# Three edits to the attention part of a mixer kernel: key products by head, queries turned by another engine, an earlier first attention product

## The chip, the cores and the metric

One core of a Trainium2 chip runs the kernel. The time is the device time of one execution, in microseconds (us); the median of three runs is given. Five engines work side by side and wait for each other by semaphores: TensorE (PE; its weight loads are shown apart as PEld), VectorE (DVE), ScalarE (ACT), GpSimd (POOL) and SyncE (SP), which issues the DMAs. Matrix products end in PSUM, which has eight banks of 2 KB in each of 128 partitions.

## The reference

Linear attention without a softmax feeds a mixer with a rotation (first mixer), which feeds a second mixer. There are 8 batches, 8 heads of 64 channels, and 576 tokens; all data are fp32.

```
kv  = einsum('bhsd,bhse->bhde', k, v)            # one 64x64 matrix per batch and head
out = einsum('bhsd,bhde->bhse', q, kv)
x   = out / sqrt(mean(out*out, -1) + 1e-6) * g_norm      # then (B, S, 512)

theta = x @ w_theta
y = w_tok_r @ (x*cos(theta)) + w_tok_i @ (x*sin(theta))  # over tokens
u = x + y
x2 = u + relu(u @ w_ch)

h = relu(x2.T @ w_tok1) @ w_tok2 ; u2 = x2 + h.T         # second mixer
out = u2 + relu(u2 @ w_ch1) @ w_ch2
```

## The kernel before

The program has four parts, one after the other: phase_a (attention and first mixer, batch by batch), and phase_b to phase_d (the second mixer). Only phase_a is touched, and one wait at the entry of phase_b. Each engine has its own hand-written list of instructions; what one engine issues it executes in that order, so a wait holds everything behind it on that engine.

Most products are made exact enough by splitting both operands into a high part (fp32r, made by ACT with a copy) and a low part (the difference, made by DVE or POOL) and adding three products: high by high, high by low, low by high (`split_matmul`, L40 to L44). The attention's own products and the transposes are plain fp32; in the trace a plain fp32 product is two pairs of a weight load and a pass, a transpose one pair.

Tokens come in five slices (four of 128, one of 64). In phase_a an engine's `body(b)` does batch b's mixer and, woven into it, batch b+1's attention. Body 0 (`first=True`) also prepares weights; bodies 1 to 6 are a loop, body 7 stands alone. On TensorE a body is, in order:

1. `theta(b, j)` for five slices (L281 on): x times w_theta, into banks that DVE empties (`fraction`, L653 on). From slice 2 on it waits until DVE has done the slice before last.
2. `kv(b+1)` (L229): for five slices and four pairs of heads one fp32 product of 128 by 128, into the bank `ps_kv`; of each only the two diagonal 64 by 64 blocks are used. DVE's `kv_copy` (L618) copies these into a block-diagonal tile (two copies), whose other blocks are zero. `kv_copy` stands on DVE after all of the batch's `fraction`, `magnitude` and `rotate`.
3. `q_transpose(b+1, 0)` (L245): four transposes of 128 by 128 of the queries, against the identity; ACT copies the bank out (`q_copy`, L469).
4. `token_mix_first_half(b)` (L352): the token products of four column groups, in five pairs of tiles (four of two, one of one). For each pair TensorE first waits for the high parts (`a_zhi`, ACT), does 16 products (8 in the last pair), then waits for the low parts (`g_zlo`, POOL's `z_lo`, L850) and does 8 (4).
5. `attend(b+1, 0)` (L257): four fp32 products of the turned queries (stationary) with the block-diagonal tile (moving), then `q_transpose(b+1, 1)`.
6. For the groups 4 to 7: `token_mix(b, g)` (27 products), `attend(b+1, g-3)`, and, but for the last, `q_transpose(b+1, g-2)`. `attend(n, j)` waits from j=2 on until DVE has done `norm(n, j-2)` (L634), because two banks take turns.
7. `channel_mix(b, g)` for eight groups (12 products each), with transposes of the new x between them (`x_transpose`, L268) and after them.

DVE meanwhile does, in its own order: `fraction`, `magnitude`, `rotate` of the five slices; `kv_copy`; for the groups 0 to 7 `residual` (two additions, L689 on), `u_lo`, and from group 3 on `mean_square` and from group 4 on `norm` of the next batch; then for the groups 0 to 7 `relu_add` (L706), with the transposes of the result (`turn_x2`, L714, 32 by 32 blocks inside 128 by 576), `norm` of slice 4 and `x_lo`. `mean_square(n, j)` waits for ACT's `squares(n, j)`, which stands behind `u_hi` on ACT. POOL raises the mean square to the power -1/2 and multiplies by g_norm (`inverse_rms`, `gain`).

SP issues in body b: `load_kv(b+2)`, which waits for kv(b+1), `load_q(b+2)` (five DMAs, rows of 256 B), which waits for the last `q_transpose` of batch b+1, the store of x2 and 16 DMAs that store the turned result in blocks of 32 by 32 (`store_turned`, rows of 128 B).

## Time and profile before

| | |
|---|---|
| time, median of 3 runs (range) | 1215.15 us (1215.12 to 1215.16) |
| the profiled execution's own time | 1213.61 us |
| its span, first to last instruction | 1211.8 us |
| granted TensorE clock, mean | 0.995 of 2.4 GHz |
| token products of phase_a on TensorE | until 553.9 us of the span |

The span leaves out 1.8 us that lie around the first and the last instruction. A row of the timeline gives the start, the length, the engine, the line of the code, the operation, what it writes and reads, the shape and the number of like instructions in a row; in brackets stands how long the engine sat idle before it and who released it. A product's length includes its way through the array, so products overlap in the rows: the pace of a series is (length of the row minus length of one) divided by (count minus 1).

### The profile page before, as it was taken

The page shows a single profiled execution, that of the slowest core. Times are in us where ns is not written, and L with a number is a line of the kernel's source. Part 1 is how long each engine was busy: PE and PEld are TensorE (multiplying, and loading weights), DVE is VectorE, ACT ScalarE, POOL GpSimd, SP SyncE. Part 2 cuts the span into 40 slices and gives each one's busy share as a digit, 9 for nine tenths or more (in the row PEclk, how much of TensorE's full clock was granted, in tenths as well). Part 3 has the DMA queues.
Part 4 walks back from the last instruction along what each step waited for, and adds up shares of the span by engine and source line. Part 5 has one row for each costly group of instructions (what it writes and reads, how often), then busy time and mean ns, then how long its engine had stood idle before and what let it go on. Part 6 is the DMA issues. An engine that isn't in the chain of part 4 may idle for free.

```text
span 1211.8 us, 20530 instructions
## 1 busy us (share of the span) xinstructions
PE 1182.7 (98%) x7590; PEld 1150.9 (95%) x7590; DVE 836.4 (69%) x1227; ACT 490.0 (40%) x764; POOL 338.2 (28%) x209
## 2 busy tenths in 40 slices
PE   6999999999999999999999899999999999999998
PEld 5899999999999999999898899999999899999998
DVE  3877778686868778678556566766766786666664
ACT  3532424242433324244433455555556543333331
POOL 4443534444252525440553042133210000000000
PEclk9999999999999999999999999999999999999999
DMA  9825445272543440036998587856669999989973
GB/s 254 172 53 112 79 94 101 39 156 39 111 76 86 78 107 10 34 87 227 344 300 295 164 332 267 298 201 263 248 233 334 382 304 300 271 240 308 290 189 53
DMA packets 348428, 228.12 MB, mean 188 GB/s; under 512 B 268880, under 2 KB 316368, under 8 KB 347344
## 3 DMA queue, kind: packets, MB, share of 16 engines
q1 hardware_dynamic: 348368, 227.32, 64.7%
q8 instruction: 38, 0.62, 0.2%
q14 instruction: 22, 0.18, 0.0%
HBM read 136.84 MB, written 92.80 MB: 189 GB/s over the span
## 4 chain that ended last, share of the span: by engine, by line
PE 91%; DMA 3%; DVE 2%; issue 1%; ACT 1%; SPq 1%; POOL 0%; DVEq 0%; POOLq 0%; ACTq 0%
PE bank L42 11%; PE bank L44 11%; PE bank L43 11%; PE bank L1267 10%; PE bank L1269 10%; PE bank L1268 10%; PE bank L309 6%; PE bank L314 6%; PE bank L308 6%; PE bank L240 3%; PE bank L265 3%; PE bank L279 1%; PE bank L253 1%; DMA attention_g<-g_scratch 1%; DMA qkv_x_tokens<-x_tokens_scratch 1%
## 5 line engine op out<-in xcount | busy, mean ns | idle before, releaser
L308 PE MATMUL bank<-weights_tok,z_z 128*128 128x288 f32 x576 | 164.2, 299 | 0.0
L309 PE MATMUL bank<-weights_tok,z_z 128*128 128x288 f32 x576 | 161.3, 295 | 0.0
L314 PE MATMUL bank<-weights_tok,z_z 128*128 128x288 f32 x576 | 124.8, 294 | 0.0
L309 PEld LDWEIGHTS bank<-weights_tok,z_z 128*128 128x128 f32 x576 | 108.2, 188 | 0.0
L308 PEld LDWEIGHTS bank<-weights_tok,z_z 128*128 128x128 f32 x576 | 108.1, 188 | 0.0
L838 POOL TENSOR_TENSOR weights_rms_inverse<-weights_mean_squares,weights_minus_half 128x8 f32<-128x8 f32 x40 | 65.5, 1639 | 129.6 <-DVE weights_mean_squares L632 129.3
L314 PEld LDWEIGHTS bank<-weights_tok,z_z 128*128 128x128 f32 x576 | 92.6, 188 | 0.0
L519 ACT ACTIVATE weights_x_channel_major<-attention_u 128x288 fp32r<-128x288 f32 x64 | 28.4, 444 | 139.4 <-DVE attention_u L699 138.8
L853 POOL TENSOR_TENSOR z_z<-tokens_cos,z_z 128x512 fp32r<-128x512 f32 x24 | 34.5, 1437 | 173.5 <-ACT z_z L512 173.5
L42 PE MATMUL bank<-weights_x_channel_major,weights_ch 128*128 128x288 f32 x256 | 77.2, 301 | 0.0
L43 PE MATMUL bank<-weights_x_channel_major,weights_ch 128*128 128x288 f32 x256 | 75.4, 294 | 0.0
L44 PE MATMUL bank<-weights_x_channel_major,weights_ch 128*128 128x288 f32 x256 | 75.4, 294 | 0.0
L1496 ACT ACTIVATE attention_staged<-bank 128x384 f32<-128x384 f32 x108 | 52.3, 489 | 36.1 <-PE bank L1269 31.3
L697 DVE TENSOR_TENSOR attention_u<-bank,weights_x_channel_major 128x288 f32<-128x288 f32 x64 | 29.1, 454 | 52.5 <-PE bank L314 52.4
L1267 PE MATMUL bank<-z_u_slot,weights_up 128*128 128x384 f32 x192 | 64.1, 334 | 0.0
L1268 PE MATMUL bank<-z_u_slot,weights_up 128*128 128x384 f32 x192 | 64.1, 334 | 0.0
L1269 PE MATMUL bank<-z_u_slot,weights_up 128*128 128x384 f32 x192 | 64.1, 334 | 0.0
L846 POOL TENSOR_TENSOR tokens_x_token_major<-attention_x_normed,weights_g_norm 128x512 f32<-128x512 f32 x40 | 52.7, 1326 | 0.0
L484 ACT ACTIVATE weights_x_channel_major<-bank 128x512 fp32r<-128x512 f32 (+1 forms) x40 | 21.6, 557 | 76.7 <-PE bank L279 76.7
L42 PE MATMUL bank<-weights_theta,weights_x_channel_major 128*128 128x512 f32 x128 | 51.0, 398 | 0.4 <-DVE weights_theta L735 0.4
L1549 DVE TENSOR_TENSOR attention_staged<-attention_staged 128x384 f32<-128x384 f32 x36 | 28.1, 781 | 32.7 <-ACT attention_staged L1496 32.5
L44 PE MATMUL bank<-weights_theta,weights_x_channel_major 128*128 128x512 f32 x128 | 50.0, 390 | 0.0
(287 smaller groups left out, 3697.7 us busy)
## 6 DMA issues: line engine op xcount, KB each, us to landing
g_scratch<-attention_staged SPq DMA_DIRECT2D x36, 960.0 KB, 5.0
weights_g<-g_scratch SPq DMA_DIRECT2D x24, 1152.0 KB, 10.3
g_scratch<-attention_staged SPq DMA_DIRECT2D x36, 384.0 KB, 5.6
x_scratch<-attention_u SPq DMA_DIRECT2D x8, 1152.0 KB, 4.5
u_scratch<-attention_u SPq DMA_DIRECT2D x8, 1152.0 KB, 6.2
weights_raw_u<-u_scratch SPq DMA_DIRECT2D x6, 1536.0 KB, 7.4
qkv_u_left<-u_scratch SPq DMA_DIRECT2D x12, 768.0 KB, 9.4
qkv_k<-in_k_dram SPq DMA_DIRECT2D x32, 256.0 KB, 4.9
```

The costliest lines, as they stand in the source:

```text
L42: eng.matmul(out, w[0], x[0], start=first, stop=False)
L43: eng.matmul(out, w[0], x[1], start=False, stop=False)
L44: return eng.matmul(out, w[1], x[0], start=False, stop=last)
L308: pe.matmul(out, x, wtok[0][:, zt, hs], start=(i == 0), stop=False)
L309: pe.matmul(out, x, wtok[1][:, zt, hs], start=False, stop=False)
L314: mm = pe.matmul(tok_bank(b, g)[:, 0:HALF], z[1][:, zt, c * P:(c + 1) * P], wtok[0][:, zt, half * HALF:(half + 1) * HALF], start=False, st ...
L838: gp.tensor_tensor(rms_inv[:, i, :], msq[:, i, :], minus_half[:, :], ALU.pow).then_inc(g_pow, 1)
L846: gp.tensor_tensor(xtm[:, j, :].rearrange("p (h e) -> p h e", h=H), xn[:, i, :].rearrange("p (h e) -> p h e", h=H), gn[:, :].unsqueeze(1). ...
L1267: eng.matmul(out, w[0], x[0], start=False, stop=False, skip_group_check=True)
L1268: eng.matmul(out, w[0], x[1], start=False, stop=False, skip_group_check=True)
L1269: return eng.matmul(out, w[1], x[0], start=False, stop=last, skip_group_check=True)
L1496: act.activation(tile(n, k), src, ACT.Relu).then_inc(done, 1)
```

## The change

- **Keys by head on column halves.** `kv` takes each head by itself: a weight load of 64 columns (k) and a product with 64 moving columns (v), even heads into partitions 0 to 63, odd heads into 64 to 127, of half as many columns of the bank. 40 fp32 products of half width take the place of 20. `kv_copy` makes four copies of 64 by 128 into two tiles, and stands on DVE behind slice 3's `magnitude` and slice 2's `rotate`, before slice 4's `fraction`.
- **Queries from batch 2 on turned by DVE.** `load_blocks` loads queries in 16 DMAs so that blocks of 32 by 32 lie in place, and `turn_q` turns them on DVE with four transposes of 128 by 576; in bodies 1 to 5 behind `relu_add` of the groups 1 to 4, in body 0 (for batch 2) at the very end of DVE's list. TensorE's `q_transpose` and ACT's `q_copy` stay for batches 0 and 1 alone. The turned queries have a tile for all five slices; `attend` reads 64 columns of it for the last slice.
- **First attention product between token pairs.** `attend(b+1, 0)` stands behind the second of the five pairs of `token_mix_first_half`, in the other of the two banks.
- In body 0 ACT's `q_copy(1, 0)` and the conversion of w_ch stand earlier. `squares` writes into a slice of `fraction`, one `x_normed` tile shares memory with `x_left`, so `sines` of slice 3 waits for the batch's last `theta`.

```diff
@@ sync
-        def load_q(n):
-            wait(sp, p_qt, NT * n)
-            for j in range(NT):
-                load_tile(qin, q, n, j, s_q)
+        def load_blocks(n):
+            if isinstance(n, int) and n == PE_TURNED:
+                sp.wait_ge(p_qt, NT * n)
+            else:
+                sp.wait_ge(d_q, HP * (n - PE_TURNED))
+            for hp in range(HP):
+                for part in range(PARTS):
+                    h, first = 2 * hp + part // 2, part % 2 * SIDE
+                    sp.dma_start(q_raw[part * SIDE:(part + 1) * SIDE, hp, :].rearrange("p (b d) -> p b d", d=SIDE),
+                                 q[n, h, :, first:first + SIDE].rearrange("(b s) d -> s b d", s=SIDE)
+                                 ).then_inc(s_q, DMA)
...
@@ tensor, kv
-                    hs = slice(2 * hp, 2 * hp + 2)
-                    mm = pe.matmul(ps_kv[:, hp * P:(hp + 1) * P], kin[:, j, hs, :].rearrange("p h d -> p (h d)"),
-                                   vin[:, j, hs, :].rearrange("p h d -> p (h d)"), start=(j == 0 and hp == 0),
-                                   stop=(j == NT - 1 and hp == HP - 1))
+                    for side in range(2):
+                        h = 2 * hp + side
+                        mm = pe.matmul(ps_kv[side * D:(side + 1) * D, hp * D:(hp + 1) * D], kin[:, j, h, :],
+                                       vin[:, j, h, :], start=(j == 0 and hp == 0),
+                                       stop=(j == NT - 1 and hp == HP - 1))
...
@@ tensor, attend
-            pe.wait_ge(a_qt, NT * n + j + 1)
-            pe.wait_ge(d_kv, 2 * (n + 1))
+            if isinstance(n, int) and n < PE_TURNED:
+                pe.wait_ge(a_qt, NT * n + j + 1)
+            else:
+                pe.wait_ge(d_q, HP * (n - PE_TURNED + 1))
+            pe.wait_ge(d_kv, 4 * (n + 1))
...
-                mm = pe.matmul(ps_out[j % 2][:, hp * P:(hp + 1) * P], qt[:, j % 2, hp, :], kvbd[:, hp, :],
-                               start=True, stop=True)
+                mm = pe.matmul(ps_out[j % 2][0:rows(j), hp * P:(hp + 1) * P], qt[:, hp, j * P:j * P + rows(j)],
+                               kvbd[hp // 2][:, hp % 2, :], start=True, stop=True)
...
@@ tensor, token_mix_first_half
                 token_mix_pair(b, pair, FIRST_HALF)
+                if pair == 1:
+                    attend(b + 1, 0)
...
@@ tensor, body
                 kv(b + 1)
-                q_transpose(b + 1, 0)
+                if first:
+                    q_transpose(b + 1, 0)
...
                 token_mix_first_half(b)
-                attend(b + 1, 0)
-                q_transpose(b + 1, 1)
+                if first:
+                    q_transpose(b + 1, 1)
                 for g in range(NC, NG):
                     token_mix(b, g)
                     attend(b + 1, g - 3)
-                    if g < NG - 1:
+                    if first and g < NG - 1:
                         q_transpose(b + 1, g - 2)
...
@@ scalar, body 0
                     z_hi(0, j)
+                    if j == 1:
+                        q_copy(1, 0)
                     if j >= 2 and j + 1 < NT:
                         sines(0, j + 1)
-                act.wait_ge(s_raw[2], DMA)
-                act.activation(wch[0][:, :, :], raw_ch[:, :, :], ACT.Copy).then_inc(a_whi, 1)
+                    if j == 2:
+                        act.wait_ge(s_raw[2], DMA)
+                        act.activation(wch[0][:, :, :], raw_ch[:, :, :], ACT.Copy).then_inc(a_whi, 1)
...
@@ vector
-            pv = ps_kv[:, :].rearrange("p (a e) -> p a e", a=HP)
-            dve.tensor_copy(kvbd[0:D, :, 0:D], pv[0:D, :, 0:D]).then_inc(d_kv, 1)
-            dve.tensor_copy(kvbd[D:P, :, D:P], pv[D:P, :, D:P]).then_inc(d_kv, 1)
+            pv = ps_kv[:, 0:HP * D].rearrange("p (a e) -> p a e", a=HP)
+            for side in range(2):
+                hs = slice(side * D, (side + 1) * D)
+                for t in range(2):
+                    dve.tensor_copy(kvbd[t][hs, :, hs], pv[hs, 2 * t:2 * t + 2, :]).then_inc(d_kv, 1)
+        def turn_q(n, hp):
+            if hp == 0:
+                dve.wait_ge(s_q, NT * DMA + HP * PARTS * DMA * (n - PE_TURNED + 1))
+                dve.wait_ge(p_out, NT * n)
+            dve.transpose(qt[:, hp, :], q_raw[:, hp, :]).then_inc(d_q, 1)
...
                     if j >= 1:
                         rotate(b, j - 1)
-            if more:
-                kv_copy(b + 1)
+                    if more and j == 3:
+                        kv_copy(b + 1)
...
                 if more and g == 0:
                     norm(b + 1, NT - 1)
+                if more and turn and not first and 1 <= g <= HP:
+                    turn_q(b + 2, g - 1)
...
                 turn_x2(b, NC - 1, turned)
+                if first:
+                    for hp in range(HP):
+                        turn_q(b + 2, hp)
...
@@ phase_b, load_first
-        sp.wait_ge(*prev["p_qt"])
+        sp.wait_ge(*prev["d_q"])
```

## Rows read from the trace of the kernel before

**Rows 1.** The page: busy time of each engine, share, count.
```profile
PE 1182.7 (98%) x7590; PEld 1150.9 (95%) x7590; DVE 836.4 (69%) x1227; ACT 490.0 (40%) x764; POOL 338.2 (28%) x209
```

**Rows 2.** Busy time by stretch; 173 to 240 us is one period (body 2 into 3).
```profile
core 0: us, PE busy (x) PEld busy (x) DVE busy (x) ACT busy (x) POOL busy (x), PEclk, DMA share, GB/s
173.00:240.00 67.00, 67.00 (x487) 64.77 (x486) 51.45 (x85) 23.28 (x44) 28.77 (x19) 1.00 0.45 88
240.00:307.00 67.00, 67.00 (x487) 64.77 (x486) 51.44 (x85) 23.56 (x44) 28.75 (x19) 1.00 0.45 88
```

**Rows 3.** Waits of TensorE over the whole span: us in total, times, longest.
```profile
PE bank L265 <- issue: 2.6, 1, 2.6
```

**Rows 4.** Timeline of TensorE, 173 to 240 us.
```profile
188.18 4.62 PE L240 MATMUL bank<-qkv_v,qkv_k 128*128 128x128 f32 x40
192.64 0.60 PE L253 MATMUL bank<-const_ident,qkv_q 128*128 128x128 f32 x4
...
201.51 1.21 PE L314 MATMUL bank<-weights_tok,z_z 128*128 128x288 f32 x8
...
204.67 1.21 PE L314 MATMUL bank<-weights_tok,z_z 128*128 128x288 f32 x8
...
207.30 1.05 PE L265 MATMUL bank<-attention_kv_blockdiag,attention_q_transposed 128*128 128x128 f32 x8
208.19 0.60 PE L253 MATMUL bank<-const_ident,qkv_q 128*128 128x128 f32 x4
...
217.16 1.05 PE L265 MATMUL bank<-attention_kv_blockdiag,attention_q_transposed 128*128 128x128 f32 x8
```

**Rows 5.** Weight loads by form; timeline of TensorE at 27.77 us (five full, four half transposes).
```profile
L393 PEld LDWEIGHTS bank<-const_ident,z_raw_tok 128*128 128x128 f32 x40 | 4.7, 140 | 1.2 <-DMA z_raw_tok<-in_moe_w_tok_r_dram 0.5
L393 PEld LDWEIGHTS bank<-const_ident,z_raw_tok 128*64 128x64 f32 x10 | 1.1, 111 | 0.0
...
27.77 1.15 PE L393 MATMUL bank<-const_ident,z_raw_tok 128*128 128x128 f32 x9
```

**Rows 6.** Timeline of DVE, 173 to 242 us.
```profile
202.43 0.42 DVE L621 COPY attention_kv_blockdiag<-bank 64x256 f32<-64x256 f32 x1
...
207.28 0.46 DVE L697 TENSOR_TENSOR attention_u<-bank,weights_x_channel_major 128x288 f32<-128x288 f32 x1 [3.97 <-PE bank L314]
...
212.54 0.17 DVE L632 TENSOR_SCALAR weights_mean_squares<-weights_sum_squares 128x8 f32<-128x8 f32 x1
...
215.49 0.69 DVE L640 TENSOR_TENSOR attention_x_normed<-bank,weights_rms_inverse 128x512 f32<-128x512 f32 x1
...
238.07 0.46 DVE L712 SCALAR_TENSOR_TENSOR attention_u<-bank,attention_u 128x288 f32<-128x288 f32 x1 [1.58 <-PE bank L44]
238.44 0.77 DVE L722 STREAM_TRANSPOSE z_x_turned<-attention_u 128x576 f32<-128x576 f32 x1
239.14 0.65 DVE L651 TENSOR_TENSOR weights_x_channel_major<-bank,weights_x_channel_major 128x512 fp32r<-128x512 f32 x1
```

**Rows 7.** Timeline of POOL, the low parts of tile pairs four and five.
```profile
201.81 1.75 POOL L855 TENSOR_TENSOR z_z<-attention_x_normed,z_z 128x512 fp32r<-128x512 f32 x1
203.51 1.30 POOL L858 TENSOR_TENSOR z_z<-tokens_cos,z_z 128x512 fp32r<-128x512 f32 x1
```

**Rows 8.** Timeline of body 0, 67 to 73 us: ACT, DVE, TensorE.
```profile
67.33 1.90 ACT L578 ACTIVATE weights_ch<-attention_raw_ch 128x2048 fp32r<-128x2048 f32 x1
...
69.27 2.29 DVE L783 TENSOR_TENSOR weights_ch<-attention_raw_ch,weights_ch 128x2048 fp32r<-128x2048 f32 x1 [2.51 <-ACT weights_ch L578]
...
72.44 1.13 PE L265 MATMUL bank<-attention_kv_blockdiag,attention_q_transposed 128*128 128x128 f32 x8 [2.56 <-issue]
```

**Rows 9.** Timeline at the start of body 1: DVE, and TensorE's third theta slice.
```profile
112.02 0.69 DVE L670 TENSOR_TENSOR weights_fraction<-bank,tokens_cos 128x512 f32<-128x512 f32 x1
...
113.53 0.39 PE L42 MATMUL bank<-weights_theta,weights_x_channel_major 128*128 128x512 f32 x1
```

**Rows 10.** Timeline of SP's DMA issues, 170 to 245 us (length: the issue).
```profile
175.51 10.61 SPq L164 DMA_DIRECT2D x_tokens_scratch<-z_x_turned  x16
...
202.16 0.61 SPq L174 DMA_DIRECT2D qkv_v<-in_v_dram  x1
```

More of the change, by code:

```diff
@@ L588, in body @@
                         z_hi(b, j - 2)
-            if more:
-                q_copy(b + 1, 0)
             for g in range(NG):
                 u_hi(b, g)
-                if more and g == 0:
+                if first and g == 0:
                     q_copy(b + 1, 1)
@@ L598, in body @@
                     squares(b + 1, g - 3)
-                    if g < NG - 1:
+                    if first and g < NG - 1:
                         q_copy(b + 1, g - 2)
@@ L760, in vector, with body @@
         norm(0, 4)
-        def body(b, first=False, more=True):
+        def body(b, first=False, more=True, turn=True):
             if first:
@@ L828, in vector @@
         body(0, first=True)
-        loop(dve, body, 1, B - 1)
+        loop(dve, body, 1, B - 2)
+        body(B - 2, turn=False)
         body(B - 1, more=False)
```

79 lines of the change are left out of this document (45 added, 34 removed).

## The prediction

> **What bounds the kernel now.** I read the busy times first: TensorE is busy 98% of the span, DVE 69%, ACT 40%, POOL 28% [rows 1]. Then the stretches: from body 1 to body 6 every period is 67.00 us, and in it TensorE is busy for the whole 67.00 at a granted clock of 1.00 (2.4 GHz), DVE for 51.45 [rows 2]. So TensorE's own work sets the length of a body, and a pass that leaves its list shortens the body as long as nobody else becomes late. The waits of TensorE come next: in the mixer bodies there is only one, 2.6 us before the attention product of body 0 [rows 3]. Last the timelines of the four engines in one period, to see how close the others are behind. They are close in two places, and these decide the forecast.
>
> **Part 1: queries turned by DVE.** Four transposes in a row take 0.60 us with the last one's 0.27 in it, so the pace is (0.60 - 0.27)/3 = 0.109 us and a group costs 0.44 [rows 4]; the array goes on without a gap afterwards. Five groups in each of bodies 1 to 6 leave: 5 x 0.44 = 2.18 us a body, 13.1 in all. ACT's copies leave too; ACT has room (23.3 of 67), I give nothing for it.
> DVE gets four transposes of 128x576. The same shape in `turn_x2` stands 0.70 from start to start (238.44 to 239.14 [rows 6]), so 2.8 us a body, behind `relu_add` of groups 1 to 4. A pass of 288 columns has the pace (1.21 - 0.29)/7 = 0.131 [rows 4], so a channel group takes TensorE 12 x 0.131 = 1.58 us, and DVE's relu and a transpose 0.40 + 0.70 = 1.10; DVE enters late by some microseconds, but has caught up at group 5, where it now waits 1.58 [rows 6]. I count 0; if the cover is gone (POOL's gain products stretching each transpose), it is up to 1.3 us a body.
> The load: 16 DMAs of the shape of `store_turned`, which SP issues in 10.6 us, against five. They stand behind the key loads, whose last is issued at 202.16 [rows 10], so they are issued by about 213.4; the first `turn_q` stands four channel groups before the relu at 238.07 [rows 6], so after 231. SP's next duty is the store of x2 at the end of the body. I count 0.
> In body 0 the four transposes stand at the end of DVE's list, where no channel group covers them. The next `fraction` ended at 112.71, and theta's third slice, which waits for it, started at 113.53 [rows 9]: 0.82 of cover against 2.8. So about +2.0 us, once.
>
> **Part 2: keys by head.** Forty pairs take 4.62 us, pace (4.62 - 0.28)/39 = 0.111 [rows 4]; now there are 80 pairs with half the columns in the load and in the pass. The trace has no pass with 64 moving columns. Bounds: if both halves cost half and neighbours on the two column halves run side by side, 80 x 0.028 = 2.2 us; if only the halving holds, 80 x 0.056 = 4.5, no change; if a pair doesn't get cheaper at all, 80 x 0.111 = 8.9. Halving the weight load's columns alone changes nothing: five full and four half transposes keep (1.15 - 0.27)/8 = 0.110 [rows 5], so there the pass with its 128 moving columns sets the pace, and here it is the pass that is halved. Between ends so far apart I take the middle of the first two, 3.4 us (-1.1 a batch), since neighbours share neither weights nor output partitions.
> The rule that speaks for the side-by-side end stands in the Trainium skill, "TensorEngine Tiling (Array Packing)", section "Key Properties": different tiles can load weights and multiply in parallel. No row here shows two tiles at once; by it the keys cost 2.2 us, and the end is the same, as the next paragraph shows.
>
> **Part 3: what is late next in the first half.** The low products of pair four started at 204.67 [rows 4], and POOL had their operand at 201.81 + 1.75 = 203.56 [rows 7]: 1.1 us of cover. TensorE now comes there earlier by 0.44 (transposes) and 1.1 (keys), later by 0.89 (eight attention passes of 0.111, moved in front): at 204.0. POOL comes later: the four copies of `kv_copy` now stand before `fraction` of slice 4 and `rotate` of slice 3. A copy of 64x256 takes 0.42, an operation on 8 elements 0.17 [rows 6]; one of 64x128 lies between, about 0.30, four 1.2. So the operand is there at up to 203.56 + 1.2 = 204.8, and TensorE waits about 0.8. The bounds: 0 (the copies fall into an idle spot) and 2.0 (keys at 2.2 us). Whatever the keys save beyond 0.3 us is thus given back here, in every body of the loop.
>
> **Part 4: what is late next in the second half.** The third attention product waits for DVE's first `norm`. That ended at 215.49 + 0.69 = 216.18, which is 8.9 us after the first half's end at 207.30 on TensorE [rows 4, 6], and TensorE came at 217.16, or 9.86: 1.0 of cover. Now TensorE has only 27 x 0.131 = 3.55, 0.89 and 3.55 to do: it comes after 8.0, while DVE starts its residuals at the same point and still needs 8.9. It waits 0.9. After that a step is 4.44 on TensorE; DVE's steps, with POOL's products in the way, are as long or longer, so I add 0.2: 1.1 a body. Bounds 0 and 2.
>
> **Part 5: body 0.** The product at 72.44 waited 2.56 us because `kv_copy` stood behind DVE's 2.29 us for the low part of w_ch, and that behind ACT's 1.90 [rows 8]. Both are moved off; but `q_copy(1, 0)` now stands on ACT before slice 3's `sines` and waits for the transposes, which makes the later tiles late, and DVE's 2.29 still precedes its residuals. I take half, -1.3 (bounds -2.6 and +0.5). At the start the first keys wait for their DMAs: 0 (bounds -1 and +0.5).
>
> **Sum.** A body of the loop: -2.18 - 1.1 + 0.8 + 1.1 = -1.4, six of them -8.4; body 0 -1.3; the end of body 0 +2.0; with -0.6 for what body 0's keys save: -8.3. On the profiled execution (1213.6, span 1211.8 and 1.8 around it) that is 1205.3. The median of the runs is 1.5 above it, so 1206.8 is my number.
>
> **Rivals.**
> *A. The keys cost what they did* (4.5 us): no wait in the first half, so a body gains 2.18 - 1.1 = 1.1: -6.5 - 1.3 + 2.0 = -5.8, 1209.4. For it: only the halving is certain.
> *B. Nobody gets late:* DVE's and POOL's chains move with TensorE. -13.1 - 7 x 1.1 - 1.3 + 2.0 = -20; with unchanged keys -12.4: 1195 to 1203. Against it: covers of 1.1 and 1.0 us, both smaller than what is removed ahead of them.
> *C. Slower: a pair of half width isn't half a pair.* If the pace falls only as the weight load's length did from 128 to 64 columns (140 to 111 ns, 0.79 [rows 5]), it is 0.088 and the keys cost 7.0 us, +2.6. Then nothing waits in the first half; a body is -2.18 + 2.6 + 1.1 = +1.5; sum 6 x 1.5 + 2.6 - 1.3 + 2.0 = +12.3: 1227. It decides from 0.066 us a pair (keys +0.8) on. At the end of no gain per pair (+4.5) it would be +26: 1241.
> The Trainium skill, "TensorE: Matmul & The Clock Gate", section "Back-to-back issue gap", speaks for C: in a stream of weight load and product the load counts too, about 81 ns per pair at 128 columns. No row shows a short pair that would test it. By it as an estimate the keys would cost 6.5 us and the kernel would take about 1223.
> *D. DVE becomes the bound:* the turned queries are stretched by 1.3 us a body, theta's start slips and the low parts with it: a body gains only 0.4, sum -2.4 - 1.3 + 2.0 = -1.7: 1213.5. For it: DVE goes from 51.45 to some 54.6 busy of 65.6.
>
> **How the numbers follow.** Forecast 0.45, A 0.20, B 0.11, C 0.13, D 0.11. Range 1199 to 1214: it leaves out C and the lower part of B. A measurement of this kernel can tell 0.2%, 2.4 us, from no change. Faster than 1212.7: forecast, A, B and a fifth of D, 0.78. Within 1212.7 to 1217.6: most of D and a slip of A, 0.09. Slower: C, 0.13.
>
> **What would show it.** The key row: 80 pairs in 2.2 to 4.1 us and no transposes of queries after body 0. Waits of TensorE that were not there: before L314 in the first half (on POOL's low part) and before the third attention product (on DVE's `norm`), each near 1 us, in every body; one of about 2 us before theta's third slice in body 1. The period should read 65.4 to 65.8 instead of 67.00. I am wrong if the key row is longer than 5.3 us, if the period is under 64.5, or if TensorE waits for `relu_add` or for queries.

## The result and the profile after

The kernel with the change takes 1205.78 us (median of 4 runs, 1204.34 to 1206.46), the one before 1215.13 in the same session (1214.69 to 1215.16). The ratio is 0.9922, 95% interval 0.9905 to 0.9939: 0.8% faster. The forecast was 1206.8.

The page of the changed kernel, busy time and share of the span:

```profile
PE 1166.1 (97%) x7790; PEld 1122.9 (93%) x7790; DVE 846.1 (70%) x1267; ACT 474.5 (39%) x734; POOL 325.1 (27%) x210
```

TensorE is busy 16.6 us less than in [rows 1], but its share fell as well: part of what left its list came back as waiting. The stretches show it (busy time of each engine, granted clock, DMA share; columns as in [rows 2]):

```profile
175.50:241.50 66.00, 64.83 (x511) 60.96 (x509) 52.30 (x93) 21.01 (x40) 26.56 (x19) 1.00 0.48 89
241.50:307.50 66.00, 64.81 (x511) 60.94 (x509) 52.33 (x92) 20.99 (x40) 26.59 (x19) 1.00 0.47 89
```

In each period 1.2 us of TensorE is idle, where before it was never idle. These stretches have the length that I gave them, so they don't measure the period. That comes from the starts of the last angle slice: 67.39 us before (186.36, 253.75, ...), 65.99 after (186.47, 252.45, ...). The forecast's "every period is 67.00" had taken the chosen length of [rows 2] for a measurement. A stretch in which an engine is always busy looks the same at any length.

The waits of TensorE in one period (total, times, longest; in the kernel before this answer had no line):

```profile
PE bank L328 <- ACT z_z L538: 0.5, 1, 0.5
PE bank L328 <- DVE attention_u L733: 0.3, 1, 0.3
PE bank L334 <- POOL z_z L899: 0.2, 1, 0.2
```

L328 and L329 are the token products with the high parts, L334 those with the low parts. TensorE waits for the high part of pair four, ahead of group 4 for the first residual, and for the low part of pair four. The timeline of TensorE has the key products (to be read against [rows 4]), the places of these waits and, last, the third attention product, ahead of which a short wait stands that the list leaves out:

```profile
188.37 2.55 PE L257 MATMUL bank<-qkv_v,qkv_k 128*64 128x64 f32 x80
190.90 0.39 PE L328 MATMUL bank<-weights_tok,z_z 128*128 128x288 f32 x1
...
200.32 1.21 PE L334 MATMUL bank<-weights_tok,z_z 128*128 128x288 f32 x8
202.04 0.40 PE L328 MATMUL bank<-weights_tok,z_z 128*128 128x288 f32 x1 [0.51 <-ACT z_z L538]
...
204.65 1.32 PE L334 MATMUL bank<-weights_tok,z_z 128*128 128x288 f32 x8 [0.24 <-POOL z_z L899]
207.89 0.40 PE L328 MATMUL bank<-weights_tok,z_z 128*128 128x288 f32 x1 [0.33 <-DVE attention_u L733]
...
216.33 0.71 PE L285 MATMUL bank<-attention_kv_blockdiag,attention_q_transposed 128*128 128x128 f32 x4
```

**A ledger of one period.** Adding up, from the timeline, the time from the first start of each kind of work to the start of the next kind gives the following for one period of each kernel that is told of here; a wait lands in the kind ahead of it. The eight products of the angles' last slice, the channel mixing, the rest of the angles, the transposes of x and the attention products make the last column; that hardly moves in sum.

| kernel | period | keys | query transposes | token products | rest |
|---|---|---|---|---|---|
| before | 67.39 | 4.46 | 1.78 | 29.04 | 32.11 |
| after | 65.99 | 2.53 | 0 | 31.26 | 32.20 |
| keys by head alone | 66.49 | 2.48 | 1.85 | 30.00 | 32.16 |
| change, full-width keys | 66.46 | 4.38 | 0 | 30.00 | 32.08 |
| change, same halves together | 66.0 | 3.20 | 0 | 30.62 | 32.2 |
| change, queries back on TensorE | 66.95 | 2.48 | 1.97 | 30.19 | 32.31 |
| change, early product back | 66.12 | 2.55 | 0 | 31.42 | 32.15 |
| change, early product and copies back | 65.19 | 2.53 | 0 | 30.49 | 32.17 |
| change, copies on ScalarE | 65.09 | 2.54 | 0 | 30.36 | 32.19 |
| the same, second product early | 64.14 | 2.53 | 0 | 29.52 | 32.09 |

By columns the keys gave 1.93 us and the transposes 1.78; waits among the same 216 token products took 2.22 back. Net -1.40 a period. Over the steps from batch 0's last angle slice to batch 7's it is -8.2 us (475.6 before, 467.4 after). A column depends on what kind of work follows it, so it is not yet the worth of an edit; the part on the prediction comes back to that.

### The profile page after: what moved, and what is told of

It is laid out like the page before. It is cut to its first block, busy times and chain, and to the rows that moved or that the text cites. A ratio compares the mean times of both kernels' runs of the same rounds, so it can differ in the third digit from the quotient of the medians.

```text
span 1204.7 us, 21049 instructions
## 1 busy us (share of the span) xinstructions
PE 1166.1 (97%) x7790; PEld 1122.9 (93%) x7790; DVE 846.1 (70%) x1267; ACT 474.5 (39%) x734; POOL 325.1 (27%) x210
## 4 chain that ended last, share of the span: by engine, by line
PE 60%; issue 16%; POOL 8%; DVE 6%; DMA 5%; SPq 2%; ACT 2%; POOLq 0%; DVEq 0%; ACTq 0%
PE bank L1311 10%; PE bank L1313 10%; PE bank L1312 10%; PE bank L42 6%; PE bank L44 6%; PE bank L43 6%; PE bank L334 3%; POOL z_z L899 3%; PE bank L328 3%; PE bank L329 3%; POOL z_z L897 3%; DMA qkv_x_tokens<-x_tokens_scratch 2%; PE bank L285 1%; SPq L179 1%; DMA attention_g<-g_scratch 1%
## 5 line engine op out<-in xcount | busy, mean ns | idle before, releaser
L328 PE MATMUL bank<-weights_tok,z_z 128*128 128x288 f32 x576 | 165.6, 302 | 5.8 <-ACT z_z L538 3.1
L329 PE MATMUL bank<-weights_tok,z_z 128*128 128x288 f32 x576 | 161.2, 294 | 0.0
L334 PE MATMUL bank<-weights_tok,z_z 128*128 128x288 f32 x576 | 125.5, 296 | 2.1 <-POOL z_z L899 1.4
L328 PEld LDWEIGHTS bank<-weights_tok,z_z 128*128 128x128 f32 x576 | 108.1, 188 | 9.6 <-ACT z_z L538 4.5
L329 PEld LDWEIGHTS bank<-weights_tok,z_z 128*128 128x128 f32 x576 | 108.2, 188 | 0.0
L334 PEld LDWEIGHTS bank<-weights_tok,z_z 128*128 128x128 f32 x576 | 92.5, 188 | 3.8 <-POOL z_z L899 2.8
L897 POOL TENSOR_TENSOR z_z<-tokens_cos,z_z 128x512 fp32r<-128x512 f32 x24 | 31.8, 1324 | 178.4 <-ACT z_z L538 178.4
L1540 ACT ACTIVATE attention_staged<-bank 128x384 f32<-128x384 f32 x108 | 52.3, 489 | 35.2 <-PE bank L1313 30.9
L42 PE MATMUL bank<-weights_theta,weights_x_channel_major 128*128 128x512 f32 x128 | 51.1, 399 | 2.4 <-DVE weights_fraction L706 2.1
L1593 DVE TENSOR_TENSOR attention_staged<-attention_staged 128x384 f32<-128x384 f32 x36 | 31.3, 870 | 30.1 <-ACT attention_staged L1540 30.0
L44 PE MATMUL bank<-weights_theta,weights_x_channel_major 128*128 128x512 f32 x128 | 49.9, 390 | 0.0
L43 PE MATMUL bank<-weights_theta,weights_x_channel_major 128*128 128x512 f32 x128 | 49.8, 389 | 0.0
```

Source lines behind the costliest of these rows:

```text
L42: eng.matmul(out, w[0], x[0], start=first, stop=False)
L43: eng.matmul(out, w[0], x[1], start=False, stop=False)
L44: return eng.matmul(out, w[1], x[0], start=False, stop=last)
L328: pe.matmul(out, x, wtok[0][:, zt, hs], start=(i == 0), stop=False)
L329: pe.matmul(out, x, wtok[1][:, zt, hs], start=False, stop=False)
L334: mm = pe.matmul(tok_bank(b, g)[:, 0:HALF], z[1][:, zt, c * P:(c + 1) * P], wtok[0][:, zt, half * HALF:(half + 1) * HALF], start=False, st ...
```

## The experiments

### What a pair of half width costs

In the first run the eight products of a token slice were issued evens first, then odds, so that neighbours mostly share the column half:

```
-                for hp in range(HP):
-                    for side in range(2):
+                for side in range(2):
+                    for hp in range(HP):
```

> Changed from the changed kernel: within a slice the keys' products of the four even heads come first (all on one column half), then those of the odd heads (the other half); same 80 pairs. Theory (a pair is cheap only because its neighbour on the other half runs beside it; most of what the keys save is given back to a wait on POOL's low parts): the 80 pairs take about 4.5 us instead of 2.55, the two waits in the first half of the token products (about 1.2 us a body together) shrink to nothing, a period goes from 66.0 to about 66.7 us, and the kernel to 1208 to 1212 us. Rival (a half-width pair costs 0.03 us in any order): the row stays at 2.55 us, the period at 66.0, the time within 1 us of the changed kernel.

1205.53 us, ratio to the kernel before 0.9916 (0.9901 to 0.9932). Its key row in the timeline:

```profile
187.92 3.27 PE L257 MATMUL bank<-qkv_v,qkv_k 128*64 128x64 f32 x80
```

The row lies between the two expectations, the period (66.0) and the time are as the rival had them, but not for its reason. In the changed kernel's trace pairs come in twos, 6 to 7 ns from start to start and 58 ns from one two to the next; here runs of 58 ns alternate with starts of 3 to 6 ns, three of them at each change of half, so the last pairs of one half still overlap the first of the other. So both things that Part 2 left open are true: a pair of half width takes half (58 ns against 111), and pairs on different halves run side by side. The keys of the change then are at Part 2's lower bound: their pace is (2.55 - 0.22)/79 = 0.029 us a pair, where 0.028 was worked out; grouped by half it is 0.039. The 0.7 us that grouping adds cost nothing: the token products wait that much less.

The second run has the 40 full-width pairs, everything else as changed:

```
-                    for side in range(2):
-                        h = 2 * hp + side
+                    hs = slice(2 * hp, 2 * hp + 2)
...
-            pv = ps_kv[:, 0:HP * D].rearrange("p (a e) -> p a e", a=HP)
+            pv = ps_kv[:, :].rearrange("p (a e) -> p a e", a=HP)
```

> Keys by pairs of heads as in the kernel before (40 pairs of full width), everything else as in the changed kernel, with four copies of the diagonal blocks. Theory (the keys' saving is mostly given back in the first half): 4.5 us for the keys, a period of about 66.6 instead of 66.0 us; at the start TensorE is busier and its clock rises before 17 us instead of at 22, worth 1.9 us; together 1208 to 1211 us. Rival (the keys' saving of 1.9 us a batch is kept): a period of 67.9 and 1217 us or more.

1210.18 us, 0.995 (0.9933 to 0.9967). The keys cost 1.85 us more, the period 0.47 (66.46, expected 66.6). So in the company of the other two edits three quarters of the keys' gain are given back.

The keys alone, put into the kernel before:

> The kernel before with the key products by head on column halves alone (two copies of 0.43 us at their old place; queries, attention product and everything else as before). Theory (keys 2.05 us shorter; the token pairs then start 2.05 us earlier and wait 0.8 us for the low part of pair three, which GpSimd ends at 200.2 us, and 0.25 us for that of pair four): period 67.39 - 1.0 = 66.4, time 1207 to 1211. Rival 1 (nothing is late): 65.3, 1201 to 1204. Rival 2 (all is given back): 67.0 to 67.4, 1213 to 1216. Start: the first product of the angles at 33.5 to 35 if the faster keys delay the start, 32.8 if not.

1211.21 us, 0.9956 (0.9941 to 0.9972), just above the range; period 66.49, expected 66.4. TensorE's one wait in a period:

```profile
PE bank L315 <- POOL z_z L856: 0.4, 1, 0.4
```

And in the timeline of GpSimd the row that it waits for, with the next:

```profile
199.65 2.67 POOL L856 TENSOR_TENSOR z_z<-tokens_sin,z_z 128x512 fp32r<-128x512 f32 x1
202.43 1.60 POOL L854 TENSOR_TENSOR z_z<-attention_x_normed,z_z 128x512 fp32r<-128x512 f32 x1
```

The low part of pair three ends at 202.32 and TensorE's product stands at 202.38. Even alone the keys give back half (0.96 of 1.98 by the ledger's columns). In the kernel before the same part was ready at 197.48 + 2.68 = 200.16 (GpSimd's timeline)

```profile
197.48 2.68 POOL L855 TENSOR_TENSOR z_z<-tokens_sin,z_z 128x512 fp32r<-128x512 f32 x1
```

and TensorE took it at 201.51 [rows 4]: a cover of 1.35 us, against 1.1 at pair four. The keys' saving is larger than either, and pair three comes first. Besides, the step over the first batch got longer here, 72.86 us against 71.29, so that over all steps 3.8 us are left; why is open.

### Where the lateness in the first half comes from

First both moves undone for batches from 2 on: the copies stand again behind the rotations, the first attention product behind the first half.

```
-                if pair == 1:
+                if pair == (1 if isinstance(b, int) and b == 0 else NT - 1):
                     attend(b + 1, 0)
...
-                    if more and j == 3:
-                        kv_copy(b + 1)
+                if more:
+                    kv_copy(b + 1)
```

> In bodies 1 to 6 the first attention product stands behind the whole first half again, and DVE's key copies behind all of the batch's rotations, as in the kernel before; keys by head and queries on DVE stay. Theory (the four copies ahead of slice 4's fraction make POOL's low parts 1.2 us late, and the attention product's old place hid TensorE's wait for DVE's first residual): the first half ends 1.8 us earlier, a period of about 64.1 instead of 66.0 us, and 1194 to 1197 us. Rival 1 (DVE's norms are the limit wherever the product stands): a period of 65.5 or more, 1203 to 1206. Rival 2 (the product ahead fills time in which TensorE would wait anyway, and moving it back adds its 0.8 us): a period of 66.4, 1208.

1203.10 us, 0.9891 (0.9871 to 0.991): 0.8 us a period better than the change, but not 1.9. Its one wait in a period:

```profile
PE bank L334 <- POOL z_z L899: 0.7, 1, 0.7
```

That is pair three again, as in the keys alone. The expectation had left it out. GpSimd's rows for that pair:

```profile
195.61 1.76 POOL L897 TENSOR_TENSOR z_z<-tokens_cos,z_z 128x512 fp32r<-128x512 f32 x1 [2.48 <-ACT z_z L538]
197.33 2.66 POOL L899 TENSOR_TENSOR z_z<-tokens_sin,z_z 128x512 fp32r<-128x512 f32 x1
```

The low part is ready at 199.99, and TensorE's products on it start at 200.05.

Then the product alone moved back, the copies left early:

> From batch 1 on the first attention product stands again behind the whole first half of the token mixing; the copies of the key products stay early on VectorE. Theory (the early copies on VectorE are what makes the rotations, and with them the third and fourth token pairs, late; the early product only fills a gap): the waits before those pairs stay, the product covers the 0.4 us wait for the first residual and adds what is left of its 0.9 us, period 66.2 to 66.5 (66.0 with the change), time 1206 to 1209. Rival (the place of the product itself costs, by standing between pairs): period as with both moved back, 65.2, time about 1203.

1208.63 us, 0.9931 (0.991 to 0.9952), period 66.1. The period is a little under the theory's range, far from the rival's. The waits in it:

```profile
PE bank L328 <- ACT z_z L538: 1.4, 1, 1.4
PE bank L334 <- POOL z_z L899: 0.2, 1, 0.2
```

The wait for pair four's high part grew from 0.5 to 1.4 by the 0.9 us that the product takes, and there is none at pair three, though no product stands ahead of it. So the product is a filler at its early place, and the early copies make the pair late. VectorE's rows show by how much. With the change:

```profile
194.50 0.27 DVE L651 COPY attention_kv_blockdiag<-bank 64x128 f32<-64x128 f32 x1
...
195.22 0.29 DVE L651 COPY weights_kv_blockdiag<-bank 64x128 f32<-64x128 f32 x1
195.54 0.68 DVE L698 TENSOR_TENSOR weights_fraction<-bank,weights_fraction 64x512 f32<-64x512 f32 x1
196.41 1.06 DVE L703 TENSOR_SCALAR tokens_cos<-weights_fraction 64x512 f32<-64x512 f32 x1 [0.19 <-DVE weights_fraction L698]
197.50 1.65 DVE L706 TENSOR_TENSOR weights_fraction<-weights_fraction,tokens_cos 64x512 f32<-64x512 f32 x1
199.19 0.42 DVE L713 TENSOR_SCALAR tokens_cos<-weights_fraction 64x512 int32<-64x512 int32 x1
199.53 0.68 DVE L721 TENSOR_TENSOR attention_x_normed<-attention_x_normed,tokens_x_token_major 128x512 f32<-128x512 f32 x1
```

With both moves undone:

```profile
194.21 0.67 DVE L698 TENSOR_TENSOR weights_fraction<-bank,weights_fraction 64x512 f32<-64x512 f32 x1
195.07 0.42 DVE L703 TENSOR_SCALAR tokens_cos<-weights_fraction 64x512 f32<-64x512 f32 x1 [0.19 <-ACT z_z L537]
195.53 0.68 DVE L706 TENSOR_TENSOR weights_fraction<-weights_fraction,tokens_cos 64x512 f32<-64x512 f32 x1
196.25 1.41 DVE L713 TENSOR_SCALAR tokens_cos<-weights_fraction 64x512 int32<-64x512 int32 x1
197.58 0.67 DVE L721 TENSOR_TENSOR attention_x_normed<-attention_x_normed,tokens_x_token_major 128x512 f32<-128x512 f32 x1
```

L721 here starts the rotation that makes pair four. The copies take 1.04 us, but the rotation is 1.95 us later. Another 0.29 is the first row's own later start, as the whole period stands later. The rest is in L703 and L706: pushed by 1.3 us they fall beside GpSimd's low parts and take 1.06 and 1.65 us instead of 0.42 and 0.68, less 0.99 that L713 no longer loses there. GpSimd's rows with the change:

```profile
195.90 1.29 POOL L897 TENSOR_TENSOR z_z<-tokens_cos,z_z 128x512 fp32r<-128x512 f32 x1 [2.47 <-ACT z_z L538]
197.15 1.46 POOL L899 TENSOR_TENSOR z_z<-tokens_sin,z_z 128x512 fp32r<-128x512 f32 x1
202.07 1.29 POOL L897 TENSOR_TENSOR z_z<-attention_x_normed,z_z 128x512 fp32r<-128x512 f32 x1 [3.46 <-ACT z_z L538]
203.32 1.28 POOL L899 TENSOR_TENSOR z_z<-tokens_x_normed,z_z 128x512 fp32r<-128x512 f32 x1
```

L706 starts at 197.50 inside GpSimd's L899, which ends at 198.61, and ends 0.54 us after it. With both moves undone it starts at 195.53, 0.08 ahead of GpSimd's L897, and takes 0.68; there it is GpSimd that takes longer, 1.76 and 2.66 us for the two parts instead of 1.29 and 1.46. The Trainium skill, "SBUF — State Buffer", section "SBUF: two separate sides", says that VectorE and GpSimd share a pair of ports as an exclusive lock, which whoever starts first (of VectorE's operations those with two inputs in SBUF, among others) holds for a whole instruction, and that the other engine stands still meanwhile. These rows agree with that in both orders: the 0.97 us that L706 loses are most of the 1.11 until GpSimd is through. So the early copies also change who stands still: with them VectorE does, and pair four comes late; without them GpSimd does, and pair three's low part is the late one. In the kernel before GpSimd took as long for it (1.76 and 2.68 us), but TensorE came later.

If the copies on VectorE are at fault, another engine should make them. In the next run ScalarE does, from batch 2 on, and the product stays early:

```
                     if j == NJ:
                         turn_left(b)
+                        if more:
+                            kv_copy(b + 1)
...
+                    act.activation(kvbd[t][hs, :, hs], pv[hs, 2 * t:2 * t + 2, :], ACT.Copy).then_inc(d_kv, 1)
```

> From batch 2 on the four copies of the key products are made by ScalarE, between its copy of the left-over turns and its rounding of the third cosine tile, in the place of VectorE; the early attention product stays. Theory (the copies' 1.2 us ahead of VectorE's last fraction is what makes pairs three and four late, and ScalarE has 1.0 us idle there): the pairs come as with late copies and the early product fills the 1.0 us wait for the low part of pair three that those left, period 64.6 to 65.0, time 1198 to 1202. Rival 1 (ScalarE has no room: the copies delay the third tile's rounding): period 65.2 to 65.8, 1203 to 1205. Rival 2 (the copies are harmless where they are): 66.0, no change.

1202.21 us, 0.988 (0.9859 to 0.9902), period 65.09: the theory's direction, and just outside its range. The first of the four copies in ScalarE's timeline:

```profile
192.02 0.27 ACT L499 ACTIVATE attention_kv_blockdiag<-bank 64x128 f32<-64x128 f32 x1
```

The one wait that TensorE has left in a period:

```profile
PE bank L328 <- DVE attention_u L744: 0.3, 1, 0.3
```

Both waits in the first half are gone but for 0.13 us at the low part of pair four, and ScalarE rounds the third tile as early as with both moves undone (rivals 1 and 2 fall); the wait for the first residual stays, and in the ledger 0.84 us are still lost against the next run.

### The residual and the norm

On top of that the second attention product was moved ahead of group 4, and the first product's squares, mean and norm one to two groups forward:

```
+                else:
+                    attend(b + 1, 1)
                 for g in range(NC, NG):
                     token_mix(b, g)
-                    attend(b + 1, g - 3)
+                    if first or g > NC:
+                        attend(b + 1, g - 3)
...
-                if more and g == 1:
+                if more and g == (1 if first else 0):
                     squares(b + 1, 0)
...
-                if more and g >= 3:
+                if more and g == (3 if first else 2):
+                    mean_square(b + 1, 0)
+                if more and not first and g == 4:
+                    norm(b + 1, 0)
+                if more and g >= 4:
                     mean_square(b + 1, g - 3)
-                if more and g >= 4:
+                if more and g >= (4 if first else 5):
                     norm(b + 1, g - 4)
```

> As the run with ScalarE's copies; besides, the second attention product stands ahead of the fifth token group, where TensorE waits 0.4 us for the first residual, and the first product's squares, mean and norm are made one to two groups earlier so that the third product does not wait for the norm. Theory (both waits, 0.4 and 0.15 us, go): period 64.1 to 64.5, time 1195.5 to 1199. Rival (the norm, which runs through the 1.64 us power on GpSimd, comes late again and the third product waits): period as with the copies alone or up to 0.5 above.

1198.08 us, 0.9852 (0.983 to 0.9875), period 64.14, as the theory had it. The list of its waits is empty, and TensorE is busy throughout, here in a stretch of one period's length:

```profile
183.80:247.95 64.15, 64.15 (x509) 60.89 (x508) 53.28 (x88) 21.87 (x44) 28.86 (x20) 1.00 0.50 92
```

### The queries

The queries were put back on TensorE, the other edits kept:

```
-            load_blocks(b + 2)
+            load_q(b + 2)
...
-                if first:
-                    q_transpose(b + 1, 0)
+                q_transpose(b + 1, 0)
```

> Only the queries are undone: all batches are loaded by token tiles and turned by TensorE and copied by ScalarE again; keys by head, early copies and early product stay. Theory (2.18 us of TensorE per batch were removed; put back they hide about 0.4 us of the wait for the first residual and 0.15 us of that for the norm): period 66.0 + 2.18 - 0.55 = 67.6, less 2 us once at the end of the first batch, time 1212 to 1215. Rival (turning on VectorE made VectorE's chain late, so that most of the 2.18 was given back): period 66.0 to 66.8, time 1204 to 1209.

1254.78 us, 1.0317 (1.0292 to 1.0342): neither expectation. This is what TensorE waits for in a period (74 us here):

```profile
PE bank L287 <- ACT attention_q_transposed L495: 5.8, 1, 5.8
```

My edit left ScalarE's copy of the first turned queries where it stood in the kernel before, behind all roundings. The early product needs that copy, and now stood on TensorE ahead of the pairs that those roundings feed. The early product is thus only possible with queries that are turned beforehand, or with their copy moved as well. With the copy moved ahead of ScalarE's rounding of the third tile:

> The queries undone as in the run before it, with ScalarE's copy of the next batch's first turned queries moved ahead of its rounding of the third cosine tile, so that the early attention product finds them. Theory (2.18 us of TensorE per batch removed, of which 0.4 us of the wait for the first residual and 0.15 us of that for the norm came back): period 67.3 to 67.8, time 1211 to 1215. Rival (the turning's removal was mostly given back): period 66.0 to 66.8, time 1204 to 1209.

1211.47 us, 0.9951 (0.9934 to 0.9969), period 66.95. The time is in the expected range, the period between the theory's and the rival's: 0.96 us above the change's, so a little over half of the 2.18 is given back to waits. The transposes now cover those ahead of group 4 and before the third attention product, and part of the one for pair four's high part (what is left in a period):

```profile
PE bank L336 <- POOL z_z L896: 0.2, 1, 0.2
PE bank L330 <- ACT z_z L538: 0.2, 1, 0.2
```

### The end of the first batch

Batch 2's four turnings of queries stand at the end of VectorE's list of batch 0. They were moved behind its channel-mixing adds 3, 4 and 6, on top of the fastest kernel so far:

```
+                if first:
+                    for hp in {3: [0], 4: [1, 2], 6: [3]}.get(g, []):
+                        turn_q(b + 2, hp)
...
-                if first:
-                    for hp in range(HP):
-                        turn_q(b + 2, hp)
```

> ScalarE's copies and the second product early, and besides the first batch's four turnings of queries for batch 2 moved from behind VectorE's last turning of its output to the idle times after its channel-mixing adds 3, 4 and 6 (1.1, 1.6 and 0.9 us there). Theory (the 2.7 us of turnings stand on the path at the end of the first batch, where TensorE waits for the fractions): the step of the first batch falls from 71.0 to 69.0-69.5, time 1.5 to 2 us under that of the run without this move (about 1196.5). Rival (the query blocks land too late for the adds): step 71 or more.

1197.24 us, 0.9841 (0.9823 to 0.9858). The step over the first batch is 69.15 us instead of 71.02; the blocks had landed in time. Three of the four turnings in VectorE's rows:

```profile
98.87 0.77 DVE L672 STREAM_TRANSPOSE attention_q_transposed<-qkv_q_blocks 128x576 f32<-128x576 f32 x1
...
100.46 1.43 DVE L672 STREAM_TRANSPOSE attention_q_transposed<-qkv_q_blocks 128x576 f32<-128x576 f32 x2
```

This version beats both kernels: 1.6% under the one before. Its gain over the run without this move is shown in the step, not in the times, whose intervals overlap.

### The start

The first product of the angles stood at 34.65 us with the change and at 32.79 before. Two causes were tried. First the clock: with the change the record of the granted clock has 2.4 GHz from 22.3 us on. Until then four transposes in a row take 1.09 us, later 0.60, so it was at its lower level, 1.2 GHz; TensorE had done five series of keys of 1.12 us with waits for loads between them. A run with dummy products against the identity, whose result is overwritten, kept TensorE busy between the first key loads:

> The changed kernel with products of the identity with itself into a bank that nobody reads: eight before the first keys, three before each of the slices 1 to 3 of batch 0's keys, one before slice 4. Theory (at the start the short key products leave TensorE so little to do that its clock stays at 1.2 GHz until 22.3 us, and that costs the start 1.9 us): the granted clock is 2.4 GHz well before 17 us, the first theta product starts at 32.8 us or before instead of 34.65, and the kernel takes about 1204 us. Rival (the start is bound by DVE, ACT and DMAs): the clock rises, but theta starts within 0.5 us of 34.65 and the time stays.

1206.08 us, 0.9917 (0.9901 to 0.9934), no gain: the clock stood at 2.4 GHz from 5.5 to 22.6 us, but the first product of the angles came at 36.53, later than both expectations. TensorE now waited 2.8 us for the raw token weights, until 22.16, and behind that wait the clock stood at 1.2 GHz until 29.4, so this run does not settle what a late clock costs. The kernel before was then profiled a second time:

> The kernel before, profiled once more, for its start. If the change's later first product (33.7 to 35.2 us in the kernels that have it, 32.8 in the profile of before) belongs to the change: 32.5 to 33.1 again. If it is the spread of single executions: 33.5 to 35.

1216.68 us, and the first product at 34.78. Its longest wait between 8 and 36 us:

```profile
PE bank L393 <- DMA z_raw_tok<-in_moe_w_tok_r_dram: 2.4, 1, 2.4
```

The first profile had 0.3 there. With the change, in all kernels but the one with dummy products, the first product came at 33.7 to 35.2 us, in the keys alone at 34.23. So single executions of the same code differ by as much as the 1.9 us, and no loss by the change is shown. That there is none is not shown either. In the ten kernels with half-width keys and no dummy products the clock first rises at 20.3 to 24.1 us, in the three profiles with full-width keys at 9.3, 11.6 and 14.9. And TensorE came to the raw weights at 21.63 with the change, without a wait, where it had waited for them until 20.51 in the first profile of before. With full-width keys and the other two edits, though, the early clock (14.9) was not worth the 1.9 us that had been expected: TensorE then waited 3.1 us for the raw weights, and the first product came at 34.79.

## Why the prediction was right, and where its steps were off

**The net was right, a body at -1.4 as forecast, and so was the mechanism: part of what TensorE loses comes back as waits in the two halves.** The transposes were sized rightly; the keys gave 0.7 us more than forecast, and waits and two costs that the forecast did not have took that back.

*Part 1, queries.* Forecast -2.18, and that is what leaves the list, though the ledger's column has 1.78. A group of transposes takes 0.355 us from its first start to the next token product's, but the product ahead of it is followed after 0.11 us by a transpose and after 0.03 by a token product, so 0.08 us more goes with each group; they stand in the columns of the keys (4.46 against 4.38 for the same full-width keys) and of the rest. The token product behind the first half shows it, before and after:

```profile
208.54 0.38 PE L308 MATMUL bank<-weights_tok,z_z 128*128 128x288 f32 x1
...
211.59 0.61 PE L285 MATMUL bank<-attention_kv_blockdiag,attention_q_transposed 128*128 128x128 f32 x4
...
212.40 0.38 PE L328 MATMUL bank<-weights_tok,z_z 128*128 128x288 f32 x1
```

From the first start of the attention product it comes after 1.24 us before (from 207.30 [rows 4] to 208.54), and behind a like product after 0.81 with the change (211.59 to 212.40): 0.43 for one group. Turning on VectorE is hidden, as forecast: four rows of 0.76 us (the timeline of VectorE, two of them)

```profile
232.16 0.77 DVE L658 STREAM_TRANSPOSE attention_q_transposed<-qkv_q_blocks 128x576 f32<-128x576 f32 x1
...
235.24 0.76 DVE L658 STREAM_TRANSPOSE attention_q_transposed<-qkv_q_blocks 128x576 f32<-128x576 f32 x1
236.79 0.46 DVE L748 SCALAR_TENSOR_TENSOR attention_u<-bank,attention_u 128x288 f32<-128x288 f32 x1 [0.79 <-PE bank L44]
```

after which VectorE still waits 0.79 us for TensorE, where it waited 1.58 in [rows 6]. At the end of body 0 TensorE waited 1.6 us for the fraction; forecast +2.0. Rival D falls. (Its gain of 0.4 a body does not follow from its 1.3 us: 1.4 less 1.3 is 0.1.)

*Part 2, keys.* This is the mis-sized term: 3.4 us taken, 2.53 measured (row length 2.55), the lower bound's mechanism. The middle of two bounds is not a nearest row. In that time are 0.20 us between the last key pair and the token product, where full-width keys have 0.03; and the first key pair starts 0.32 us after the last angle product's start instead of 0.23. So the keys are worth 4.38 - 2.53 - 0.09 = 1.76 us; forecast 1.1. Rivals A and C fall. The rule of the Trainium skill on tiles that work in parallel ("TensorEngine Tiling (Array Packing)", "Key Properties") agrees with the trace: starts 6 to 7 ns apart on different halves. The figure of the Trainium skill in "TensorE: Matmul & The Clock Gate", "Back-to-back issue gap", about 81 ns per pair at 128 columns, doesn't carry over to these pairs of 64: 58 ns on the same half, 29 ns on alternating ones.

*Part 3, the first half.* Forecast 0.8 us of waiting, measured 0.67 for the high and 0.40 for the low part of pair four (gaps between starts of 0.80 and 0.53 us, less the pace of 0.13). The low part was there at 203.32 + 1.28 = 204.60; forecast 204.8. That these agree is partly luck. Before, GpSimd made the low parts of pairs three and four without a break, in 1.59 to 2.68 us each; with the change it stood idle for 3.46 us until ScalarE had the high part, and then took 1.29 and 1.28. The lateness came through the rotation and the high part, at which TensorE first stopped and which my working did not follow; pair three, which I had left out, becomes the late one when the copies are moved back. That "whatever the keys save beyond 0.3 us is given back" holds for the most part: in the pair of runs with full and halved keys 0.47 of 1.85 us remains.

*Part 4, the second half.* Forecast 1.1, measured 0.75: 0.50 ahead of group 4 for the first residual, 0.25 before the third attention product. The norm ended at 216.28, 8.9 us after the residuals' start, exactly as worked out. I let TensorE start group 4 at once. It had done so before only since an attention product and a transpose stood there; without them it waits for the residual itself, and by that comes later to the norm. Rival B, nobody late, falls for this kernel; the run with the second product early shows that it can be had.

*A cost that no part had.* The last slice's attention product now loads 64 columns, like the keys, and TensorE's passage into and out of it takes longer:

```profile
225.51 0.65 PE L285 MATMUL bank<-attention_kv_blockdiag,attention_q_transposed 128*64 128x128 f32 x4
...
226.53 0.40 PE L42 MATMUL bank<-weights_x_channel_major,weights_ch 128*128 128x288 f32 x1
```

Its first pair starts 0.22 us after the last token product's start instead of 0.13, and the channel product 0.20 us after its last pair's instead of 0.03: with the slower pace of that product's first step 0.28 us a period.

*Part 5.* The step over body 0 is 70.97 against 71.29; with the 1.6 us at its end taken off, body 0 gained 1.9 (forecast -1.3 and -0.6). The wait of 2.56 us is gone; two new ones of 0.9 and 0.7 stand in its first half. The start: forecast 0, and within the spread of single executions.

*The sum.* A period, put together again: -2.18 for the transposes, -1.76 for the keys, +1.82 of waits (0.67, 0.40, 0.50 and 0.25), +0.42 because the product behind each of these waits is followed only after 0.21 to 0.24 us instead of 0.11 to 0.13, and +0.28 for the last slice: -1.4. The forecast had -2.18, -1.1, +0.8 and +1.1. Its own remark that cheaper keys leave the end the same was right; that the rest meets to 0.05 us is luck. The forecast added -8.3 to a profiled execution of 1213.6 and then 1.5 for the median. The steps gave -8.2: -0.3 over body 0, where +0.1 was forecast, and -7.9 over the six that follow, where -8.4 was; the last of them (batch 6 to 7) is 66.47 us long. The medians differ by 9.35; the 1.15 beyond the steps are not placed, and are no more than single executions differ by: after the last angle slice the span goes on for 687.7 us with the change, and for 688.5 and 689.6 in the two profiles of before.

## What to carry to other kernels

When TensorE is busy all the time and work is taken from its list, look at every operand that the following products wait for, high and low parts, pair by pair, not only at the one that seems tightest: here the covers were 1.0 to 1.35 us, and of 3.9 us taken off the list 1.4 were kept. An instruction that is moved forward on an engine costs its length and what it does to those behind it: 1.04 us of copies made VectorE's rotation 1.66 us later (1.95 less the 0.29 of the whole period), as the next operations fell beside GpSimd's. And a table of times by kind of work books a gap to the kind ahead of it: compare marks that both kernels have, before a term is called wrong. A piece of work that seems to be in the way (a transpose, an attention product) may be the cover of a wait; small independent products are best put where the waits are.

## What the hardware showed that was not expected

- Plain fp32 products of 64 columns on alternating column halves: 80 pairs in 2.55 us, 29 ns a pair by the pace, against 111 ns for a full-width pair; grouped by half, 3.27 us.
- The passage from full-width products to these 64-column products and back costs 0.26 us in a period at the keys (0.32 and 0.20 us between starts instead of 0.23 and 0.03), and as much at the last slice's attention product. The transposes of the raw weights change from 128 to 64 columns without it (0.11 us throughout).
- VectorE and GpSimd hold each other up, and who starts first decides which one: the same four operations of GpSimd took 1.76, 2.66, 1.58 and 1.73 us when VectorE's came first, and 1.29, 1.46, 1.29 and 1.28 us when VectorE's came later.
- In the two fastest kernels, and in that with ScalarE's copies, one step (of batch 5 to 6) is 2.3 us longer than its neighbours: VectorE stands still for 3 us at the exit of its loop (432.6 to 435.4 us in the run with the second product early) and TensorE waits 2.1 us for a fraction. With the change itself the same exit shows no such stop; there and in most other runs the step of batch 6 to 7 is 0.5 to 1.7 us longer. What causes either stays open.
